# Attention with a gated MLP on one core: the batch loop's turn, the last pair's values and the early MLP products change places

## The chip, the cores and the metric

The kernel runs on one core of a Trainium2 chip. The metric is the device time of one execution in microseconds (us). The time before is the median of three executions.

## What is computed

Four batches, eight heads, 576 positions, head size 64. Queries and keys are rotated by position, each query's softmax over all 576 keys weights the values, and the heads side by side form `x` of 576 x 512. A gated MLP with a convolution over three neighbouring positions follows:

```python
q_rot, k_rot = rotate(q), rotate(k)
scores = scale * np.matmul(q_rot, k_rot.transpose(0, 1, 3, 2))
attn = np.exp(scores - np.max(scores, axis=-1, keepdims=True))
attn = attn / (np.sum(attn, axis=-1, keepdims=True) + 1e-09)
x = heads_side_by_side(np.matmul(attn, v))        # 4 x 576 x 512
h = np.maximum(x @ w_in, 0.0)                     # 4 x 576 x 1024
conv_out = sum(conv_w[k] * shifted(h, k) for k in range(3))
y = (h * sigmoid(conv_out)) @ w_out               # 4 x 576 x 512
```

## The kernel before

Every engine has its own instruction stream, written out by hand, and the streams meet only at semaphores. Each stream has the same frame: a prologue, `attention(0)`, a hardware loop over `b` = 0, 1, 2 whose body is `gated_mlp(b)` and then `attention(b + 1)`, and behind the loop `gated_mlp(3)`. So the loop is entered once by falling into it, turns (jumps back) twice and is left once: four places where attention hands over to the MLP.

**Attention.** Heads go in four pairs. A pair has nine score tiles of 128 query rows (the fifth, i = 4, holds the 64 last rows of both heads), so a batch has 36 tiles t = 0 to 35; the first six are made at the end of the previous MLP. For a tile TensorE writes two halves of 288 scores into PSUM (L337, L338; L332 to L335 for the tail tile), VectorE takes the negated row maximum (L603), ScalarE the exponential with the row sum (L469) into `P`. Tiles go in groups of 2, 2, 1, 2, 2: GpSimd adds epsilon to the group's row sums (L773), VectorE takes the reciprocals (L620), GpSimd multiplies each tile of `P` by them (L752, "normalise"), VectorE transposes it in blocks of 32 into `turned` (L628, "turn"). When all nine tiles of a pair are turned, `times_v` (L365) multiplies by the values in 18 steps of 16 matmuls, cut into five chunks. In the trace each chunk's matmuls stand as L365: 64 records for four steps, 96 for the last six of pair 2, 288 for a whole pair. For pairs 0 to 2 the chunks lie between score tiles of the next pair; the last chunk of pair 2 comes right behind tile 35. The result of a pair lies in four PSUM banks, which ScalarE and VectorE split into a high and a low part (`x_hi` L479, `x_lo` L633). They must be split before the next pair's values may be written there.

**The end of attention before.** On TensorE: `early_hidden` for n = 0 to 3, each nine matmuls (three of the four slices of `x`, which hold pairs 0 to 2; L381 to L383), then the five chunks of the last pair's values, then the loop's turn. ScalarE and VectorE split the last pair at the end of `attention`, ahead of the turn.

**The MLP.** 16 units (two halves of positions, eight slices of 128 hidden features). Unit n: 12 matmuls on TensorE (three where the early part is done), ReLU on ScalarE (L485), first tap (L491), two taps on VectorE (L639), sigmoid (L496), gate (L647), high part (L502), low part on GpSimd (L756), and five units later 12 output matmuls (L397 to L399). A unit's PSUM bank is that of unit n - 4, so `hidden_tile(n)` waits for gate n - 4 from n = 4 on. Beside it VectorE and ScalarE rotate queries and keys of the next batch, whose loads the SyncE queue (SP) issues when the last pair's values are done: V for the next batch's second pair (L256), then `xc` and `xs` (L235, L236). VectorE's first operation on them (L584) stands ahead of its taps of unit 2, so these wait with it. In batch 0 GpSimd also makes the low halves of the weights between tiles (L762), eight times.

VectorE's stream in attention, at tile t: maximum of t, turn of t - 4, reciprocals of the group that ends with tile t - 1. The stretch t = 36 to 39 has only turns, the last reciprocals and the split of pair 2.

Of the kernel before, what the change touches and what calls it, by code (L numbers as in the profile page):

```python
# [5 lines left out]
def rope_attention_conv_gated_mlp(nc, qk, qk_swapped, v_rows, cos_table, sin_table, q_scale,  # L6
# [12 lines left out]
    B, H, _, S = qk.shape  # L19
    D = 64  # L20
    PAIRS = H // 2
    DM, FF = w_in.shape[0] * w_in.shape[1], w_in.shape[2]
    KD = DM // 128
# [12 lines left out]
    AHEAD = FULL + 2  # L36
    NB = S // 32
    BEHIND = 4
    CHUNKS = [(0, 4), (4, 8), (8, 12), (12, 15), (15, NB)]

    ctx = ExitStack()
    with ctx:
# [144 lines left out]
        def tile_at(t):  # L187
            return t // TILES, t % TILES
# [132 lines left out]
        def _(pe):  # L321
# [31 lines left out]
            def times_v(b, pair, chunk):  # L353

                if chunk == 0:
                    pe.wait_ge(turned_done, b * N_SCORES + TILES * (pair + 1))
                    pe.wait_ge(v_in[pair % 2], b * 32 + 16 * (pair // 2 + 1))
                    if pair > 0:
                        pe.wait_ge(x_split, b * PAIRS + pair)
                for k in range(*CHUNKS[chunk]):  # L360
                    for a in range(4):
                        rows = slice(32 * a, 32 * a + 32)
                        for n in range(2):
                            tiles, cols = turned_of(pair, n, a)
                            last = nc.tensor.matmul(banks[n * D:(n + 1) * D, PV0 + a, cols], V[rows, pair % 2, n, k, :],  # L365
                                                    turned[rows, tiles, 32 * k:32 * k + 32],
                                                    start=(k == 0), stop=(k == NB - 1))
                if chunk == len(CHUNKS) - 1:
                    last.then_inc(pv_done, 1)

            def hidden_tile(b, n, ks):


                half, f = n // NF, n % NF
                if n >= 4:
                    pe.wait_ge(gated, b * UNITS + (n - 3))
                cols = slice(half * HALF, half * HALF + HALO)
                fc = slice(f * 128, (f + 1) * 128)
                out = banks[:, n % 4, 0:HALO]
                for k in ks:  # L380
                    nc.tensor.matmul(out, wi_hi[:, k, fc], x_hi[:, k, cols], start=(k == 0), stop=False)  # L381
                    nc.tensor.matmul(out, wi_hi[:, k, fc], x_lo[:, k, cols], start=False, stop=False)  # L382
                    last = nc.tensor.matmul(out, wi_lo[:, k, fc], x_hi[:, k, cols], start=False,  # L383
                                            stop=(k == KD - 1))
                if ks[-1] == KD - 1:
                    last.then_inc(hidden, 1)
# [16 lines left out]
            def attention(b):  # L403
                for t in range(AHEAD, N_SCORES):
                    score(b, *tile_at(t))
                    for pair in range(PAIRS - 1):
                        for chunk in range(len(CHUNKS)):
                            if t == values_at(pair, chunk):
                                times_v(b, pair, chunk)
                for n in range(4):  # L410
                    early_hidden(b, n)
                for chunk in range(len(CHUNKS)):
                    times_v(b, PAIRS - 1, chunk)

            def gated_mlp(b, last):
                pe.wait_ge(x_split, b * PAIRS + PAIRS)
                for n in range(UNITS + LAG):
                    if n < UNITS:
                        hidden_tile(b, n, range(KD) if n >= 4 else range(KD - 1, KD))
                    if n >= LAG:  # L420
                        output_step(b, n - LAG)
                    if not last and UNITS <= n < UNITS + 2:

                        pe.wait_ge(gated, b * UNITS + (UNITS - 2 if n == UNITS else UNITS))
                        score(b + 1, *FIRST_TILES[n - UNITS])
                if not last:
                    for tile in FIRST_TILES[2:]:
                        score(b + 1, *tile)
                    pe.wait_ge(y_copied, 2 * b + 2)

            def early_hidden(b, n):

                pe.wait_ge(exps, b * N_SCORES + N_SCORES - (n < 2))
                if n == 0:
                    pe.wait_ge(x_split, b * PAIRS + (PAIRS - 1))
                    pe.wait_ge(padded, 2)
                    if isinstance(b, int) and b == 0:
                        pe.wait_ge(w_split, H // 2)
                hidden_tile(b, n, range(KD - 1))

            pe.wait_ge(kl_zeroed, 2)
            for tile in FIRST_TILES:
                score(0, *tile)
            attention(0)
            pe.wait_ge(w_split, H)
            with pe.Fori(0, B - 1) as b:
                gated_mlp(b, False)
                attention(b + 1)
            gated_mlp(B - 1, True)


        @block.scalar
        def _(act):
# [56 lines left out]
            def attention(b, first):  # L510
                for t in range(AHEAD - 1, N_SCORES):
                    exp_tile(b, *tile_at(t))
                    for pair in range(PAIRS - 1):
                        if t == values_in(pair):
                            x_high(b, pair)
                    if first and t in WEIGHTS_AT:
                        weights_high(WEIGHTS_AT.index(t))
                load_table(ACT.Sigmoid)
                x_high(b, PAIRS - 1)

            def gated_mlp(b, last):
                for n in range(UNITS + 2):
# [35 lines left out]
            act.wait_ge(rope_lo, H)  # L558
            attention(0, True)
            with act.Fori(0, B - 1) as b:  # L560
                gated_mlp(b, False)
                attention(b + 1, False)
            gated_mlp(B - 1, True)


        @block.vector
        def _(dve):
# [82 lines left out]
            def attention(b):  # L650
                turn(b, 0)
                turn(b, 1)
                for t in range(AHEAD, N_SCORES + BEHIND):
                    if t < N_SCORES:
                        max_tile(b, *tile_at(t))
                    turn(b, t - BEHIND)
                    pair, i = tile_at(t - 1)
                    for k, (_, e) in enumerate(GROUPS):
                        if pair < PAIRS and i == e - 1 and (pair > 0 or k > 2):
                            reciprocals(b, pair, k)  # L660
                    pair, i = tile_at(t)
                    if i == TILES - 1 and pair + 1 < PAIRS:
                        set_tails(b, pair + 1)
                    for pair in range(PAIRS - 1):
                        if t == values_in(pair) + 2:
                            x_low(b, pair)
                x_low(b, PAIRS - 1)

            def gated_mlp(b, last):
                for n in range(UNITS + 2):  # L670
# [59 lines left out]
            dve.wait_ge(consts_in, N_CONSTS)  # L730
            attention(0)
            with dve.Fori(0, B - 1) as b:
                gated_mlp(b, False)
                attention(b + 1)
            gated_mlp(B - 1, True)


# [112 lines left out]
```

## Time and profile before

| | us |
|---|---|
| median of three runs | 601.92 |
| the three runs | 600.47, 601.92, 605.8 |
| the profiled execution, device time | 601.05 |
| its span, first to last instruction | 599.2 |
| TensorE busy | 462.8 (77%) |
| VectorE busy | 421.6 (70%) |
| ScalarE busy | 280.2 (47%) |
| GpSimd busy | 201.0 (34%) |
| TensorE's mean granted clock | 0.906 |

Times in a timeline count from the span's start. A row gives start, duration, engine, line, operation, output and inputs, how many instructions it merges, and in brackets how long the engine stood idle before and what ended that. "issue" is idle time that ends with nothing the profile shows. A clock of 1.00 is 2.4 GHz, 0.50 is 1.2 GHz.

### The profile page before, as it was taken

How to read it: one execution, taken by the hardware profiler on the slowest of the kernel's cores; microseconds unless marked ns; L12 is line 12 of the kernel's file. 1: busy time of each engine (PE TensorE's matmuls, PEld its weight loads, DVE VectorE, ACT ScalarE, POOL GpSimd, SP SyncE). 2: the span in 40 equal slices, each digit the busy share in tenths (PEclk: the TensorE clock that was granted, in tenths of full speed). 3: DMA queues.
4: the chain of work that ended last, by engine and by line, in shares of the span. 5: the costliest groups of instructions: out<-in, count | busy, mean ns of one | idle time of the engine just before them, and what ended most of it. 6: DMA issues, size and time to landing. Idle time of an engine off the chain costs nothing.

```text
span 599.2 us, 17374 instructions
## 1 busy us (share of the span) xinstructions
PE 462.8 (77%) x6784; PEld 414.5 (69%) x6784; DVE 421.6 (70%) x796; ACT 280.2 (47%) x655; POOL 201.0 (34%) x277
## 2 busy tenths in 40 slices
PE   0054868785998698776998699875999698886996
PEld 0043656685998476575998577675999476675996
DVE  6967588707986978815997987824996987834441
ACT  1233555504666445514666453514676454525552
POOL 5312676701321244501431244511432244411321
PEclk9999968888999689987999697986999687988999
DMA  5888122204556111224567110224467101200011
GB/s 197 245 243 269 78 81 81 68 16 166 172 162 178 38 34 61 82 79 156 158 170 184 42 48 38 81 81 164 138 179 186 51 12 73 82 3 1 2 40 40
DMA packets 24370, 62.59 MB, mean 104 GB/s; under 512 B 3296, under 2 KB 7392, under 8 KB 21984
## 3 DMA queue, kind: packets, MB, share of 16 engines
q1 hardware_dynamic: 24288, 61.43, 33.0%
q8 instruction: 59, 0.97, 0.7%
q14 instruction: 23, 0.19, 0.1%
HBM read 42.55 MB, written 4.72 MB: 79 GB/s over the span
## 4 chain that ended last, share of the span: by engine, by line
PE 59%; DVE 13%; issue 13%; DMA 7%; ACT 3%; SPq 2%; POOL 1%; DVEq 1%; ACTq 0%; POOLq 0%
PE banks L365 15%; PE banks L381 6%; PE banks L382 6%; PE banks L383 6%; PE banks L337 6%; PE banks L397 5%; PE banks L399 5%; PE banks L398 5%; DVE neg_max L603 4%; PE banks L338 3%; DVE turned L628 3%; DMA Q<-K 2%; DMA xs<-qk_swapped_dram 2%; DMA KL<-Q 2%; DVE x_lo L633 2%
## 5 line engine op out<-in xcount | busy, mean ns | idle before, releaser
L469 ACT ACTIVATE P<-banks,neg_max 128x576 f32<-128x576 f32 x144 | 106.9, 742 | 132.9 <-DVE neg_max L603 131.3
L337 PE MATMUL banks<-K,Q 128*128 128x288 f32 x256 | 98.5, 395 | 81.1 <-ACT P L469 47.7
L337 PEld LDWEIGHTS banks<-K,Q 128*128 128x128 f32 x256 | 58.6, 229 | 108.7 <-ACT P L469 62.2
L603 DVE TENSOR_REDUCE neg_max<-banks 128x1 f32<-128x576 f32 x144 | 107.2, 747 | 36.2 <-PE banks L338 26.5
L756 POOL TENSOR_TENSOR u_lo<-u,u_hi 128x288 fp32r<-128x288 f32 x64 | 61.1, 956 | 201.5 <-ACT u_hi L502 201.5
L752 POOL TENSOR_SCALAR P<-P,recip 128x576 f32<-128x576 f32 x124 | 91.5, 748 | 69.2 <-DVE recip L620 69.2
L381 PE MATMUL banks<-x_hi,wi_hi 128*128 128x290 f32 x256 | 84.4, 330 | 37.3 <-DVE u L647 12.9
L628 DVE STREAM_TRANSPOSE turned<-P 128x576 f32<-128x576 f32 x144 | 109.5, 765 | 4.1 <-PE banks L365 3.7
L365 PE MATMUL banks<-turned,V 32*64 32x160 f32 (+1 forms) x4608 | 101.2, 303 | 3.6 <-issue 3.6
L639 DVE SCALAR_TENSOR_TENSOR conv<-banks,taps,conv 128x288 f32<-128x288 f32 x128 | 65.7, 514 | 46.0 <-ACT conv L491 45.8
L365 PEld LDWEIGHTS banks<-turned,V 32*64 32x64 f32 x4608 | 81.7, 136 | 15.6 <-issue 15.3
L338 PE MATMUL banks<-KL,Q 128*128 128x288 f32 x256 | 85.0, 342 | 0.0
L381 PEld LDWEIGHTS banks<-x_hi,wi_hi 128*128 128x128 f32 x256 | 54.4, 213 | 41.5 <-DVE u L647 14.6
L382 PE MATMUL banks<-x_lo,wi_hi 128*128 128x290 f32 x256 | 82.2, 321 | 0.0
L383 PE MATMUL banks<-x_hi,wi_lo 128*128 128x290 f32 x256 | 82.1, 321 | 0.0
L397 PE MATMUL banks<-u_hi,wo_hi 128*128 128x288 f32 x256 | 75.9, 296 | 0.0
L398 PE MATMUL banks<-u_lo,wo_hi 128*128 128x288 f32 x256 | 75.7, 296 | 0.0
L399 PE MATMUL banks<-u_hi,wo_lo 128*128 128x288 f32 x256 | 75.7, 296 | 0.0
L338 PEld LDWEIGHTS banks<-KL,Q 128*128 128x128 f32 x256 | 60.4, 236 | 0.0
L382 PEld LDWEIGHTS banks<-x_lo,wi_hi 128*128 128x128 f32 x256 | 54.7, 214 | 0.0
L383 PEld LDWEIGHTS banks<-x_hi,wi_lo 128*128 128x128 f32 x256 | 54.4, 212 | 0.0
L633 DVE TENSOR_TENSOR x_lo<-banks,x_hi 64x64 fp32r<-64x64 f32 (+1 forms) x48 | 16.3, 367 | 51.0 <-ACT x_hi L479 50.8
(50 smaller groups left out, 651.8 us busy)
## 6 DMA issues: line engine op xcount, KB each, us to landing
V<-v_rows_dram SPq DMA_DIRECT2D x16, 1152.0 KB, 5.1
xc<-qk_dram SPq DMA_DIRECT2D x28, 288.0 KB, 2.9
xs<-qk_swapped_dram SPq DMA_DIRECT2D x28, 288.0 KB, 4.2
KL<-Q SPq DMA_DIRECT2D x32, 144.0 KB, 3.6
Q<-K SPq DMA_DIRECT2D x32, 144.0 KB, 3.6
K<-K SPq DMA_DIRECT2D x32, 144.0 KB, 2.6
y_dram<-y_sb SPq DMA_DIRECT2D x8, 576.0 KB, 3.4
wi_raw<-w_in_dram SPq DMA_DIRECT2D x1, 2048.0 KB, 7.8
```

The costliest lines, as they stand in the source:

```text
L337: nc.tensor.matmul(out, Q[:, h, qc], K[:, h, cols], start=True, stop=False)
L338: last = nc.tensor.matmul(out, Q[:, h, qc], KL[:, h, cols], start=False, stop=True)
L365: last = nc.tensor.matmul(banks[n * D:(n + 1) * D, PV0 + a, cols], V[rows, pair % 2, n, k, :], turned[rows, tiles, 32 * k:32 * k + 32], st ...
L381: nc.tensor.matmul(out, wi_hi[:, k, fc], x_hi[:, k, cols], start=(k == 0), stop=False)
L382: nc.tensor.matmul(out, wi_hi[:, k, fc], x_lo[:, k, cols], start=False, stop=False)
L383: last = nc.tensor.matmul(out, wi_lo[:, k, fc], x_hi[:, k, cols], start=False, stop=(k == KD - 1))
L397: nc.tensor.matmul(out, wo_hi[:, f, dc], u_hi[:, n % UR, :], start=(f == 0), stop=False)
L398: nc.tensor.matmul(out, wo_hi[:, f, dc], u_lo[:, n % UR, :], start=False, stop=False)
L399: last = nc.tensor.matmul(out, wo_lo[:, f, dc], u_hi[:, n % UR, :], start=False, stop=(f == NF - 1))
L469: nc.scalar.activation(dst, src, ACT.Exp, bias=neg_max[:, c:c + 1], scale=1.0, accum_out=row_sum[:, c:c + 1]).then_inc(exps, 1)
L603: nc.vector.tensor_reduce(out=neg_max[:, c:c + 1], in_=banks[:, 2 * (t % 2):2 * (t % 2) + 2, 0:HALF], axis=AX.XY, op=ALU.max, negate=True) ...
L628: nc.vector.transpose(turned[:, turned_slot(pair, i), :], p_tile(pair, i)).then_inc(turned_done, 1)
```

## The change

Four edits. The last pair's values move on TensorE out of `attention` into a new function `last_values`, which runs behind the loop's turn and ahead of the early products; there are two of these instead of four (`EARLY = 2`), so n = 2 and 3 are made whole in the MLP. The split of the last pair (`x_high`, `x_low`) moves behind the turn too on ScalarE and VectorE. TensorE's wait for all split weights moves from ahead of the loop into `early_hidden`. On VectorE a group's reciprocals move from behind the turn at the tile after the group's end to behind the maximum of the tile after that; those of the last group stay where they were.

```diff
+    EARLY = 2
@@ tensor
-                for n in range(4):
-                    early_hidden(b, n)
+
+            def last_values(b):
                 for chunk in range(len(CHUNKS)):
                     times_v(b, PAIRS - 1, chunk)
+                for n in range(EARLY):
+                    early_hidden(b, n)
...
-                        hidden_tile(b, n, range(KD) if n >= 4 else range(KD - 1, KD))
+                        hidden_tile(b, n, range(KD) if n >= EARLY else range(KD - 1, KD))
...
                     pe.wait_ge(x_split, b * PAIRS + (PAIRS - 1))
                     pe.wait_ge(padded, 2)
-                    if isinstance(b, int) and b == 0:
-                        pe.wait_ge(w_split, H // 2)
+                    pe.wait_ge(w_split, H)
                 hidden_tile(b, n, range(KD - 1))
...
             attention(0)
-            pe.wait_ge(w_split, H)
             with pe.Fori(0, B - 1) as b:
+                last_values(b)
                 gated_mlp(b, False)
                 attention(b + 1)
+            last_values(B - 1)
             gated_mlp(B - 1, True)
@@ scalar
                 load_table(ACT.Sigmoid)
-                x_high(b, PAIRS - 1)
...
             with act.Fori(0, B - 1) as b:
+                x_high(b, PAIRS - 1)
                 gated_mlp(b, False)
                 attention(b + 1, False)
+            x_high(B - 1, PAIRS - 1)
             gated_mlp(B - 1, True)
@@ vector
                     if t < N_SCORES:
                         max_tile(b, *tile_at(t))
+                    if t == N_SCORES:
+                        turn(b, t - BEHIND)
+                        reciprocals(b, PAIRS - 1, len(GROUPS) - 1)
+                        continue
+                    pair, i = tile_at(t - 2)
+                    for k, (_, e) in enumerate(GROUPS):
+                        if t < N_SCORES and i == e - 1 and (pair > 0 or k > 2):
+                            reciprocals(b, pair, k)
                     turn(b, t - BEHIND)
-                    pair, i = tile_at(t - 1)
-                    for k, (_, e) in enumerate(GROUPS):
-                        if pair < PAIRS and i == e - 1 and (pair > 0 or k > 2):
-                            reciprocals(b, pair, k)
...
-                x_low(b, PAIRS - 1)
...
             with dve.Fori(0, B - 1) as b:
+                x_low(b, PAIRS - 1)
                 gated_mlp(b, False)
                 attention(b + 1)
+            x_low(B - 1, PAIRS - 1)
             gated_mlp(B - 1, True)
```

## Rows read from the trace of the kernel before

**Rows 1.** The page: TensorE's busy time, and the chain that ended last.

```profile
PE 462.8 (77%) x6784; PEld 414.5 (69%) x6784; DVE 421.6 (70%) x796; ACT 280.2 (47%) x655; POOL 201.0 (34%) x277
PE 59%; DVE 13%; issue 13%; DMA 7%; ACT 3%; SPq 2%; POOL 1%; DVEq 1%; ACTq 0%; POOLq 0%
```

**Rows 2.** Timeline, end of batch 1's attention: start, duration, engine, line, work, [idle before].

```profile
250.79 1.91 PE L365 MATMUL banks<-turned,V 32*64 32x160 f32 x96
...
253.48 0.12 DVE L620 RECIPROCAL recip<-recip 128x2 f32<-128x2 f32 x1
...
253.81 1.47 POOL L752 TENSOR_SCALAR P<-P,recip 128x576 f32<-128x576 f32 x2 [0.72 <-DVE recip L620]
254.20 1.02 DVE L633 TENSOR_TENSOR x_lo<-banks,x_hi 128x512 fp32r<-128x512 f32 x3
...
255.25 1.44 DVE L628 STREAM_TRANSPOSE turned<-P 128x576 f32<-128x576 f32 x2
```

**Rows 3.** The same timeline: early products, last values, first turn of the loop.

```profile
255.28 0.61 PE L381 MATMUL banks<-x_hi,wi_hi 128*128 128x290 f32 x1 [2.58 <-DVE x_lo L633]
...
261.58 4.32 PE L365 MATMUL banks<-turned,V 32*64 32x160 f32 x238
266.80 1.24 PE L365 MATMUL banks<-turned,V 32*64 32x160 f32 x50 [0.89 <-issue]
...
272.10 0.60 PE L381 MATMUL banks<-x_hi,wi_hi 128*128 128x290 f32 x1 [4.06 <-issue]
...
273.22 0.40 ACT L485 ACTIVATE banks<-banks 128x290 f32<-128x290 f32 x1 [4.21 <-PE banks L383]
```

**Rows 4.** Timelines: the loop's entry (batch 0), second turn, and exit.

```profile
119.51 1.44 DVE L628 STREAM_TRANSPOSE turned<-P 128x576 f32<-128x576 f32 x2
...
133.48 0.94 ACT L479 ACTIVATE x_hi<-banks 128x512 fp32r<-128x512 f32 x3 [15.24 <-PE banks L365]
...
136.27 0.40 ACT L485 ACTIVATE banks<-banks 128x290 f32<-128x290 f32 x1 [1.85 <-PE banks L383]
...
410.29 0.40 ACT L485 ACTIVATE banks<-banks 128x290 f32<-128x290 f32 x1 [4.67 <-PE banks L383]
...
543.95 0.40 ACT L485 ACTIVATE banks<-banks 128x290 f32<-128x290 f32 x1 [1.85 <-PE banks L383]
```

**Rows 5.** Timeline of ScalarE: the copy that ends each batch's MLP.

```profile
191.36 1.13 ACT L508 ACTIVATE y_sb<-banks 128x1152 f32<-128x1152 f32 x1 [1.17 <-PE banks L399]
...
326.59 1.13 ACT L508 ACTIVATE y_sb<-banks 128x1152 f32<-128x1152 f32 x1 [1.17 <-PE banks L399]
...
463.00 1.13 ACT L508 ACTIVATE y_sb<-banks 128x1152 f32<-128x1152 f32 x1 [1.17 <-PE banks L399]
...
594.31 1.13 ACT L508 ACTIVATE y_sb<-banks 128x1152 f32<-128x1152 f32 x1 [5.60 <-PE banks L399]
```

**Rows 6.** Timelines: the MLP's start behind the entry and behind the exit.

```profile
142.07 1.13 DVE L584 TENSOR_TENSOR xc<-xc,cos_t 128x576 f32<-128x576 f32 x1 [1.56 <-DMA xs<-qk_swapped_dram]
...
144.72 0.41 PE L381 MATMUL banks<-x_hi,wi_hi 128*128 128x290 f32 x1 [2.71 <-DVE u L647]
...
547.83 0.40 PE L381 MATMUL banks<-x_hi,wi_hi 128*128 128x290 f32 x1 [2.70 <-DVE u L647]
```

**Rows 7.** Stages: length, TensorE busy, granted clock, DMA share, GB/s.

```profile
254.00:258.00 4.00, 2.73 (x11) 0.60 0.83 292
119.00:125.00 6.00, 5.42 (x22) 0.50 0.24 101
```

**Rows 8.** Timeline of TensorE: one chunk of values at either clock.

```profile
363.59 2.44 PE L365 MATMUL banks<-turned,V 32*64 32x160 f32 x64
...
369.32 1.37 PE L365 MATMUL banks<-turned,V 32*64 32x160 f32 x64
```

**Rows 9.** Timeline of VectorE in a steady stretch: a maximum, a single tile's reciprocal.

```profile
245.17 0.73 DVE L603 TENSOR_REDUCE neg_max<-banks 128x1 f32<-128x576 f32 x1
...
247.26 0.16 DVE L620 RECIPROCAL recip<-recip 128x1 f32<-128x1 f32 x1 [0.68 <-POOL recip L773]
```

## Prediction, made before the changed kernel ran

> **What bounds the kernel now.** I read the page first: TensorE is busy 77% of the span and carries 59% of the chain that ended last, VectorE 13%, and another 13% is "issue" [rows 1]. So no engine is the bound throughout, and a change of order can only win what TensorE stands idle for on the chain. I then went through the timeline at the four places where attention hands over to the MLP, because the diff moves work there and nowhere else but in VectorE's place for the reciprocals.
>
> Batch 1 shows the pattern. The values of pair 2 end at 250.79 + 1.91 = 252.70. TensorE then stands 2.58 us until pair 2 is split by VectorE (254.20 + 1.02), does 36 early matmuls up to 261.5, writes the last values from 261.58 to 268.04, and stands 4.06 us to 272.10 [rows 2, 3]. What the last values need was there long before: tile 35 is turned at 255.25 + 1.44 = 256.69, and pair 2 split at 255.22 [rows 2]. Of the 4.06 us, some 2.1 are the split of the last pair (0.94 on ScalarE, 1.05 on VectorE, as at the entry [rows 4]); the rest is the loop's turn, since at entry and exit ReLU 0 follows the end of the values by 2.8 us (133.48, where ScalarE starts on them, to 136.27 at the entry), at the turn by 5.2 us (268.04 to 273.22) [rows 3, 4]. The turn thus holds TensorE for at least 4.06 us, of which about 2 lay behind the split.
>
> Behind each hand-over TensorE starves again: it has only short remainders of units 0 to 3 to do and then waits 2.70 us for the gate of unit 1 [rows 6]. The granted clock drops to its lower level (1.2 GHz) after such idle stretches: its mean is 0.60 from 254 to 258 and 0.50 from 119 to 125, each behind an idle wait at the end of pair 2's values [rows 7].
>
> **The change, part by part.** I add up for each hand-over the time up to ReLU 0, and then how long the MLP lasts from ReLU 0 to the copy that ends it.
>
> *A, reciprocals later.* At tile 35 the reciprocals of tiles 32 and 33 now stand behind the maximum of 35, which starts just as the chunk at 250.79 does: 251.65 in place of about 250.2. GpSimd answers 0.33 us after a reciprocal (253.48 to 253.81) and takes 1.47 for two tiles [rows 2], so it is done with 33 at 253.45, and the last epsilon, the last reciprocal (253.85), and the last two normalised tiles (255.65) follow; with turn 33, the split of 1.02 and two turns of 0.72 behind each other VectorE ends at 257.2: 0.5 us later than now. In batch 0 GpSimd also has a weight slice between tiles 32 and 33 and is on the chain throughout; there the whole shift of about 1.6 us goes through, and tile 35 is turned at 119.51 + 1.44 + 1.6 = 122.55 [rows 4]. In the steady stretches I cost the move at nothing. The cover: a reciprocal and the turn that needs it are parted by one turn (0.77) and one maximum (0.73), 1.50 us, and the way through GpSimd takes 0.33 + 0.74 = 1.07 [rows 2, 9]; 0.43 us is spare. The wait of 0.68 us for a single tile's epsilon [rows 9] stays, but then holds a turn and not a maximum; it lies in a stretch where the value chunks set TensorE's pace, so I take no gain.
>
> *B, values straight after the turn.* TensorE reaches the jump at about 252.3 and is ready 4.1 to 4.6 us later, at 256.4 to 256.9. The values can start at 257.3. So the turn is hidden, by the wait for tile 35; the margin is 0.4 to 0.9 us. ScalarE, VectorE and GpSimd jump while nothing needs them for 8 us. The values start 4.3 us earlier than now (261.58), although TensorE's idle time before them grows from 2.58 to 4.6 us.
>
> *C, their length.* Now 6.46 us with one "issue" gap of 0.89 in it [rows 3]. They will meet the low clock that the early products meet now. A chunk takes 2.44 at the low and 1.37 at the full clock [rows 8]; three low microseconds cost 1.4, the entry's five and more cost 2.4. I take 1.8. Directly behind the jump the instruction stream may be thin; of this the rows show only the gap of 0.89 with work in hand and the 4.06 of the jump. I take 0.3 us more at the two turns, near the former, since TensorE waits for tile 35 anyhow, and keep 4.06 for the range.
>
> *D, from the values' end to ReLU 0.* The split of the last pair (0.94 + 1.05 and two hand-offs, 2.1 us) is now covered by 18 early matmuls. A matmul takes (594.31 - 547.83 - 1.6 for a low stretch) / 336 = 0.133 us [rows 5, 6], so they last 2.4, and with the three that finish unit 0 ReLU 0 comes 2.85 after the values. At entry and exit that is what it is now; at the turns it is 5.2 now.
>
> So ReLU 0 comes
> - entry: 122.65 + 6.46 + 1.8 + 2.85 = 133.8, now 136.27: -2.5
> - turns: 257.3 + 6.46 + 1.8 + 0.3 + 2.85 = 268.7, now 273.22: -4.5 each (I take the second like the first)
> - exit: as a turn without the 0.3, against a present without the jump, 268.04 + 2.8: -2.4
>
> *E, the MLP.* From ReLU 0 to the closing copy it takes 55.1 us behind the entry, 53.4 and 52.7 behind the turns and 50.4 behind the exit [rows 3, 4, 5]. Units 2 and 3 are now made whole: 18 matmuls more, 2.4 us, which fit into the 2.70 us of idle time ahead of gate 1 [rows 6]. At the exit that also keeps the clock up: TensorE has 363 matmuls, 48.4 us, and about 0.4 of waiting, in place of 50.4: -1.5. At the entry the tables of the next batch decide. The loads are issued when the values end and land 8.6 us later, at 142.07, with VectorE waiting 1.56 us, and TensorE then 2.71 for gate 2 [rows 4, 6]. That is counted from the values' end, so it stays at the entry. At the turns it is hidden today behind the 5.2 us; with 2.85 in its place the turns get the entry's start. Their MLP becomes 55.1: +1.7 and +2.4. This is the chief giving back.
>
> Sum: entry -2.5; first turn -4.5 + 1.7 = -2.8; second -4.5 + 2.4 = -2.1; exit -2.4 - 1.5 = -3.9. Together -11.3 on the profiled execution's 601.05: 589.8. The median of the runs is 0.9 above that execution, so I say 590.
>
> **The rivals.**
> - *Cheaper start.* The loads land in time at the turns, as they do now, and the low clock costs the lower bound of 1.4. For it: the transfer has the memory to itself there. Against: the entry's row. It gives another 4.1 + 4 x 0.4 = 5.7 us: 584.
> - *The jump starves the values.* They are the densest instruction stream in the kernel: 288 matmuls in 5.6 us, while the MLP, on which the jump falls now, has 12 in 1.6. If a second fetch like the first is exposed inside them, each turn loses 4.06: 8.1 in all, 598. For it: a gap of 0.89 occurs even in straight code, and the load of V is issued in the same moment as the jump. Against: the 0.3 to 0.9 us of waiting and the low clock give the stream time. The Trainium skill, "Runtime: NRT & Kernel Launch", section Instruction fetch mechanics, says that a taken branch breaks the sequential prefetch and forces a fetch before execution can go on; the 4.06 us [rows 3] agree with it, and by that rule the next blocks too would have to come in while the values run.
> - *Slower: the later reciprocals stall VectorE.* If a turn comes to wait for its normalised tile, it is 0.3 us (the 0.73 of the maximum less the spare 0.43) for each of some 16 groups of a batch, 64 in all: +19, so 609 with nothing gained and about 598 with the rest as forecast. It decides once GpSimd's way exceeds 1.50 us. In steady stretches it takes 1.07. In batch 0 with its weights it can happen, eight times at most.
> - *It does nothing.* TensorE could be so bound in the MLP that what is won ahead of it is lost inside. Against it: at the exit nothing stands between MLP and end, and 2.70 us of idle time are there to be filled.
>
> **Chances.** Forecast 0.52 (its own range 587 to 593); cheaper start 0.21; starved values 0.17, mostly in part, 593 to 598; stalls of VectorE 0.05; nothing 0.05. One per cent, 6 us, is about what a measurement of this kernel can tell from no change. Below 595.9 lie the first two and nearly half of the third: 0.81. Slower by over 1% only the fourth with the gains lost: 0.03. The range of 8 in 10 goes from the cheaper start to the starved values: 583.5 to 597.
>
> **What would show it.** In the profile after: the values of the last pair start about 0.1 us behind turn 35 and at most 5 us behind pair 2's values (B); their length is 8 to 9 us with a low clock at their start (C); ReLU 0 comes 2.85 us after them at all four places (D); VectorE's first table product waits 1 to 2 us for a load behind each turn, and TensorE's wait for gate 1 is nearly gone (E); spacing of the maxima in steady stretches unchanged (A). Wrong would be: "issue" gaps of together more than 2 us inside the values at the turns, turns that wait for GpSimd in batches 1 to 3, or no load wait behind the turns.

## The result and the profile after

The changed kernel takes 577.5 us (575.2 to 579.8 in four runs) against 602.2 (the three runs known before and a fourth), a ratio of 0.960 (0.956 to 0.965). The gain is 24.7 us. The direction was forecast; the size was about twice the forecast 12, and 577.5 lies below the range. The profiled execution has a span of 575.7 against 599.2 us. Its page: TensorE's busy time, the chain, and the granted clock in 40 slices:

```profile
PE 456.1 (79%) x6784; PEld 407.9 (71%) x6784; DVE 419.3 (73%) x796; ACT 280.5 (49%) x655; POOL 202.7 (35%) x277
...
PEclk9999979779999597979999597889999789889999
...
PE 51%; DVE 18%; issue 12%; DMA 7%; POOL 4%; ACT 4%; SPq 2%; DVEq 0%; POOLq 0%; ACTq 0%
```

TensorE's work is the same 6784 matmuls, and its busy time fell by 6.7 us [rows 1], since less of it ran at the low clock (96.0 us of the span in place of 112.6 in the two profiled executions). The timeline of the end of batch 1's attention, against [rows 2, 3] (start, duration, engine, line, work, idle time before):

```profile
243.59 1.91 PE L366 MATMUL banks<-turned,V 32*64 32x160 f32 x96
243.70 0.76 DVE L607 TENSOR_REDUCE neg_max<-banks 128x1 f32<-128x576 f32 x1 [0.58 <-PE banks L339]
244.38 0.16 DVE L624 RECIPROCAL recip<-recip 128x2 f32<-128x2 f32 x1
...
247.34 1.02 DVE L637 TENSOR_TENSOR x_lo<-banks,x_hi 128x512 fp32r<-128x512 f32 x3
...
248.39 1.44 DVE L632 STREAM_TRANSPOSE turned<-P 128x576 f32<-128x576 f32 x2
```

```profile
250.10 6.14 PE L366 MATMUL banks<-turned,V 32*64 32x160 f32 x216 [4.60 <-DVE turned L632]
256.63 1.59 PE L366 MATMUL banks<-turned,V 32*64 32x128 f32 x72 [0.39 <-issue]
258.15 0.40 PE L382 MATMUL banks<-x_hi,wi_hi 128*128 128x290 f32 x1
...
259.25 1.06 DVE L637 TENSOR_TENSOR x_lo<-banks,x_hi 128x512 fp32r<-128x512 f32 x3 [9.42 <-ACT x_hi L482]
...
261.26 0.40 ACT L488 ACTIVATE banks<-banks 128x290 f32<-128x290 f32 x1 [2.04 <-PE banks L384]
```

TensorE waits 4.60 us, and what ends that wait is the turned tile 35 (ready at 249.83) and not the jump: at the exit, where no jump lies, it waits 4.38. The loop's turn is no longer on the path. The wait of 4.06 us [rows 3] is gone, and the split of the last pair at 259.25 lies beside early products. The MLP begins 15.8 us behind the end of pair 2's values in place of 20.5.

The copies that end the MLPs, against [rows 5]:

```profile
182.83 1.13 ACT L511 ACTIVATE y_sb<-banks 128x1152 f32<-128x1152 f32 x1 [1.17 <-PE banks L400]
...
312.78 1.13 ACT L511 ACTIVATE y_sb<-banks 128x1152 f32<-128x1152 f32 x1 [1.17 <-PE banks L400]
...
443.77 1.13 ACT L511 ACTIVATE y_sb<-banks 128x1152 f32<-128x1152 f32 x1 [1.18 <-PE banks L400]
...
570.88 1.13 ACT L511 ACTIVATE y_sb<-banks 128x1152 f32<-128x1152 f32 x1 [5.60 <-PE banks L400]
```

The same marks (start of the span or the copy before, the end of pair 2's values, ReLU 0, the closing copy) cut both traces into stages. Lengths in us, before to after; the last column is what the prediction said of the difference:

| stage | batch 0 | batch 1 | batch 2 | batch 3 | sum | predicted |
|---|---|---|---|---|---|---|
| attention up to pair 2's values | 115.7 to 114.1 | 61.3 to 62.7 | 62.6 to 64.1 | 62.7 to 62.8 | +1.4 | 0 |
| from there to ReLU 0 | 20.6 to 17.1 | 20.5 to 15.8 | 21.1 to 15.0 | 18.3 to 14.9 | -17.8 | -13.9 |
| MLP, ReLU 0 to the copy | 55.1 to 51.7 | 53.4 to 51.5 | 52.7 to 51.9 | 50.4 to 49.4 | -7.0 | +2.6 |

The third line holds most of what was missed: 9.6 of 12 us. Two views show what became of it. The clock and TensorE's load in the four MLPs, before and then after (length, busy times, granted clock, DMA share, GB/s):

```profile
136.30:191.20 54.90, 49.15 (x355) 48.44 (x353) 44.92 (x84) 33.68 (x79) 15.24 (x16) 0.97 0.57 171
273.30:326.40 53.10, 49.90 (x354) 48.93 (x354) 45.25 (x84) 33.61 (x79) 16.59 (x16) 0.95 0.55 159
410.30:462.80 52.50, 50.29 (x354) 49.57 (x354) 44.55 (x84) 33.71 (x79) 16.43 (x16) 0.92 0.55 157
544.00:594.20 50.20, 47.50 (x345) 47.09 (x343) 21.11 (x48) 25.06 (x65) 12.88 (x16) 0.97 0.04 13
```

```profile
131.20:182.70 51.50, 50.07 (x373) 49.37 (x372) 44.55 (x84) 33.77 (x79) 16.54 (x16) 1.00 0.60 180
261.30:312.60 51.30, 50.00 (x372) 49.30 (x371) 44.46 (x84) 33.74 (x79) 16.50 (x16) 1.00 0.60 179
391.90:443.60 51.70, 50.38 (x372) 49.44 (x371) 45.11 (x84) 33.61 (x79) 15.97 (x16) 1.00 0.60 178
521.50:570.80 49.30, 48.71 (x363) 48.05 (x361) 21.12 (x48) 25.05 (x65) 12.87 (x16) 1.00 0.04 13
```

All four MLPs now run at 2.4 GHz throughout; before, each had low stretches. With 18 more matmuls in each, TensorE is busy nearly all the time. And VectorE's first table product behind the turn, against [rows 6]:

```profile
265.00 0.51 DVE L643 SCALAR_TENSOR_TENSOR conv<-banks,taps,conv 128x288 f32<-128x288 f32 x1
265.42 0.75 DVE L588 TENSOR_TENSOR xc<-xc,cos_t 128x576 f32<-128x576 f32 x1
```

It follows its predecessor without a gap (0.04 us at the entry). The load wait that the prediction set at three places did not come at any.

### The profile page after: what moved, and what is told of

It reads as the page before. It is cut to its first block, busy times and chain, and to the rows that moved or that the text cites. A ratio compares the mean times of both kernels' runs of the same rounds, so it can differ in the third digit from the quotient of the medians.

```text
span 575.7 us, 17377 instructions
## 1 busy us (share of the span) xinstructions
PE 456.1 (79%) x6784; PEld 407.9 (71%) x6784; DVE 419.3 (73%) x796; ACT 280.5 (49%) x655; POOL 202.7 (35%) x277
## 4 chain that ended last, share of the span: by engine, by line
PE 51%; DVE 18%; issue 12%; DMA 7%; POOL 4%; ACT 4%; SPq 2%; DVEq 0%; POOLq 0%; ACTq 0%
PE banks L366 15%; PE banks L338 6%; DVE neg_max L607 5%; PE banks L398 4%; PE banks L400 4%; PE banks L399 4%; PE banks L382 4%; PE banks L384 4%; PE banks L383 4%; DVE turned L632 3%; PE banks L339 3%; DVE conv L643 3%; DMA Q<-K 2%; DMA xs<-qk_swapped_dram 2%; DVE xs L592 2%
## 5 line engine op out<-in xcount | busy, mean ns | idle before, releaser
L366 PE MATMUL banks<-turned,V 32*64 32x128 f32 (+1 forms) x4608 | 109.9, 322 | 21.6 <-DVE turned L632 20.4
L366 PEld LDWEIGHTS banks<-turned,V 32*64 32x64 f32 x4608 | 90.3, 146 | 33.9 <-issue 29.2
L382 PE MATMUL banks<-x_hi,wi_hi 128*128 128x290 f32 x256 | 77.0, 301 | 3.6 <-DVE u L651 3.6
L384 PE MATMUL banks<-x_hi,wi_lo 128*128 128x290 f32 x256 | 76.0, 297 | 0.0
L383 PE MATMUL banks<-x_lo,wi_hi 128*128 128x290 f32 x256 | 75.9, 297 | 0.0
L382 PEld LDWEIGHTS banks<-x_hi,wi_hi 128*128 128x128 f32 x256 | 48.4, 189 | 6.4 <-DVE u L651 5.5
L384 PEld LDWEIGHTS banks<-x_hi,wi_lo 128*128 128x128 f32 x256 | 48.3, 189 | 0.0
L398 PEld LDWEIGHTS banks<-u_hi,wo_hi 128*128 128x128 f32 x256 | 48.1, 188 | 0.3 <-ACT y_sb L511 0.3
L383 PEld LDWEIGHTS banks<-x_lo,wi_hi 128*128 128x128 f32 x256 | 48.2, 188 | 0.0
```

Of the source, the lines that this page charges most:

```text
L398: nc.tensor.matmul(out, wo_hi[:, f, dc], u_hi[:, n % UR, :], start=(f == 0), stop=False)
```

## Experiments

In the order of the questions: which part carries the gain, whether the load wait is real, and what decides whether it comes.

**The reciprocals alone.** The kernel before with

```diff
-                    turn(b, t - BEHIND)
-                    ... reciprocals of the group that ends with t - 1
+                    ... reciprocals of the group that ends with t - 2
+                    turn(b, t - BEHIND)
```

> The kernel before with the later reciprocals alone. By the prediction (steady stretches unchanged, tile 35 turned 1.6 us later in batch 0 and 0.5 us later in each other batch) it takes about 603 to 605 us against 602. By the theory formed from the trace after (in batch 0 a wait for GpSimd now falls behind a maximum that used to be held up by it, so pair 2 of batch 0 ends 1.6 us earlier, and the rest is as predicted) it takes 600 to 602 us. If the reciprocals carry a large part of the 24 us gained, it takes under 597 us.

Measured: ratio 1.0015 to before (0.998 to 1.005), 602.9 us. No gain and no loss beyond the measurement, which does not tell the first two ranges apart.

**The change without the reciprocals.** The reverse edit on the changed kernel.

> The changed kernel with the reciprocals where they were before. By the prediction it gains 2 to 3 us more than the change: about 575 us. By the theory from the trace after it loses what batch 0 gained: 577.5 to 580 us. Read beside the reciprocals alone: where both differences agree in size, the two parts add up.

Measured: 577.8 us, ratio 0.960 (0.957 to 0.964). Again nothing. The traces show why the sum is about zero. With the late reciprocals pair 2 of batch 0 ends at 114.09 in place of 116.94 us. Over all traces it ends at 112.8 to 115.1 us in the seven traces with the late reciprocals and at 114.4 to 118.8 in the seven with the old ones, 2.4 us apart in the mean. What the traces show as the reason: a maximum now runs ahead of VectorE's wait for a row sum from GpSimd, which is busy with a weight slice; before, it stood behind it (first two lines after, last two before):

```profile
68.84 0.76 DVE L607 TENSOR_REDUCE neg_max<-banks 128x1 f32<-128x576 f32 x1
72.38 0.17 DVE L624 RECIPROCAL recip<-recip 128x1 f32<-128x1 f32 x1 [2.78 <-POOL recip L782]
...
71.80 0.16 DVE L620 RECIPROCAL recip<-recip 128x1 f32<-128x1 f32 x1 [3.02 <-POOL recip L773]
71.88 0.74 DVE L603 TENSOR_REDUCE neg_max<-banks 128x1 f32<-128x576 f32 x1
```

But tile 35 is turned 6.60 us behind it in place of 5.25, and 4.32 in place of 3.99 in the other batches, 2.3 us in all. The prediction had the second half (1.6 and 0.5 us) and not the first.

**Four early products, behind the values.** The changed kernel with

```diff
-    EARLY = 2
+    EARLY = 4
```

> The changed kernel with all four early products behind the last values. If the idle time ahead of gate 1 is what the two whole units fill, ReLU 0 comes 2.4 us later at each of four places and that idle time is back: at least 577.5 + 4 x 2.4 = 587 us, and up to 4 x 1.7 = 7 us more if the granted clock falls in it again (594). If the gain lies in the order alone (values in the wait for the turned tiles), the number of early products does not matter: 578 us. In the profile the first wait of the matmuls of unit 4 is 2.5 us by the first, 0.3 us by the second.

Measured: 588.5 us, ratio 0.978 (0.974 to 0.981). ReLU 0 comes 5.45 to 5.49 us behind the values in place of 3.04 to 3.06, and TensorE again waits for gate 1 (timeline of TensorE behind the first turn):

```profile
272.46 0.40 PE L382 MATMUL banks<-x_hi,wi_hi 128*128 128x290 f32 x1 [2.71 <-DVE u L651]
```

So with the values first, 11 of the 24.7 us hang on the number of early products: what stands behind the values should be as long as the split of the last pair, and the rest fills the wait for gate 1. In the traces 9.7 us lie between the values and ReLU 0. The MLPs, with that wait and 3.4 us of low clock behind it but no load wait, are only 0.4 to 1.0 us longer each.

**The loop's turn alone.** The kernel before, with its order of early products and values kept, but the jump ahead of both and the splits of the last pair behind it on ScalarE and VectorE.

```diff
             with pe.Fori(0, B - 1) as b:
+                last_values(b)      # in this run: four early products, then the values
                 gated_mlp(b, False)
                 attention(b + 1)
```

> The kernel before with the loop's turn ahead of the four early products and the last values, which keep their old order, and the old reciprocals. If the turn's cost of about 2 us behind the split is what is won, it gains 2 x 2.3 = 4.6 us: 597.5 us. If the jump of more than 4 us only takes the place of the 2.58 us wait ahead of the early products, 1.5 to 2 us of that are given back at each of two turns: 600 to 602 us. A gain of 10 us or more would say that the turn is the change.

Measured: 602.8 us, ratio 1.004 (1.000 to 1.008). The early products behind the jump start after 3.46 us of waiting in place of 2.58, and ReLU 0 at the turns comes 2.9 and 3.3 us behind the values, as forecast in D; yet nothing is won. At the first turn the hand-over is no shorter (20.4 us in place of 20.5), since the longer wait is followed by more low clock, in which the early products take 7.5 us in place of 6.3; at the second it is 1.0 us shorter. The MLPs behind the turns are 1.7 and 1.9 us longer, with the following line (VectorE behind the first turn):

```profile
280.94 1.23 DVE L588 TENSOR_TENSOR xc<-xc,cos_t 128x576 f32<-128x576 f32 x1 [1.46 <-DMA xs<-qk_swapped_dram]
```

Here is the load wait that the prediction expected at the turns: 1.46 and 0.89 us, and MLPs of 55.1 and 54.7 us. The prediction's step E described this kernel rightly, and not the one that was forecast.

**The order and the number, without the jump's move.** The kernel before, values ahead of two early products, everything inside `attention`, the jump behind, the old reciprocals.

```diff
+    EARLY = 2
...
-                for n in range(4):
-                    early_hidden(b, n)
                 for chunk in range(len(CHUNKS)):
                     times_v(b, PAIRS - 1, chunk)
+                for n in range(EARLY):
+                    early_hidden(b, n)
...
-                        hidden_tile(b, n, range(KD) if n >= 4 else range(KD - 1, KD))
+                        hidden_tile(b, n, range(KD) if n >= EARLY else range(KD - 1, KD))
```

> The kernel before with the last values ahead of two early products, all of it still inside attention, so that the loop turns behind them; the old reciprocals. Everything of the change but the turn's place and the reciprocals. If the order carries the gain, it takes 577.5 + 2 x 2 (the jump of 4 us is shared between the split's 2 us, which the two early products cover, and the rest) to 577.5 + 2 x 4.3 (the jump lies bare) = 581.5 to 586 us. By the prediction's terms, in which the load wait gives back 4 us at the turns that a bare jump would hide, about 592 us.

Measured: 584.7 us, ratio 0.970 (0.962 to 0.978). The order and the number together bring 17 of 24.7 us without the jump's move. The order alone, with four early products, stands in two runs with the jump ahead (they differ in the reciprocals too, which bring nothing): 602.8 us with the early products first, 588.5 with the values first. Two early products in the old order were not run. In this run the jump is only half bare, TensorE waits 1.29 us for it and 1.74 us for gate 1:

```profile
252.49 6.63 PE L366 MATMUL banks<-turned,V 32*64 32x160 f32 x275 [4.13 <-DVE turned L629]
...
264.08 0.39 PE L382 MATMUL banks<-x_hi,wi_hi 128*128 128x290 f32 x1 [1.29 <-issue]
270.08 0.40 PE L382 MATMUL banks<-x_hi,wi_hi 128*128 128x290 f32 x1 [1.74 <-DVE u L648]
```

Moving the jump ahead of the values brings the other 7, although it brings nothing in the old order.

**Is the load wait behind the entry real?** The kernel before, once more.

> The kernel before once more, for its trace. The prediction took a wait of 1.56 us for a load behind the entry for a fixed price. If it is fixed, VectorE again waits over 1 us there for the load and the MLP behind the entry again takes 55 us from its first ReLU to the closing copy. If it was one execution's accident, the wait is under 0.5 us and the MLP takes about 53 us.

Measured: 602.3 us in one run; VectorE waits 1.55 us (1.56 in [rows 6]), and the MLP behind the entry takes 55.1 us again.

```profile
143.38 1.14 DVE L584 TENSOR_TENSOR xc<-xc,cos_t 128x576 f32<-128x576 f32 x1 [1.55 <-DMA xs<-qk_swapped_dram]
```

It is no accident of one execution.

**The tables' loads first, in both kernels.**

```diff
-                load_v(b + 1, 1)
                 prepare(b + 1)      # its first two heads' loads
+                                    # load_v follows them
```

> The kernel before with the loads of the first two heads' tables of the next batch issued ahead of the load of V. They then land some 2.5 us earlier. If the load wait behind the entry is real and costs what the prediction says, the entry gains 1.6 us of wait and up to 1.7 us of low clock: 599 to 600 us against 602. At the turns nothing changes. If it was an accident: 602 us.

Measured: ratio 0.995 (0.991 to 0.999), 600.3 us. The wait is gone (the load lands 4.2 us behind the values in place of 8.6), and the MLP behind the entry takes 51.8 us in place of 55.1:

```profile
144.12 0.75 DVE L585 TENSOR_TENSOR xc<-xc,cos_t 128x576 f32<-128x576 f32 x1
```

In that stage the wait's price is that of the prediction, 1.6 us plus what follows it, 3.3 together. What follows is the low clock, and 0.4 us by which the product behind the wait is slower (1.13 in [rows 6], 0.75 here). The whole kernel gains 3.2 us by the ratio (0.9 to 5.6), 1.8 by the medians. Against the expectation the MLPs behind the turns are shorter too, 51.9 and 52.0 us; their waits for the load had been 0.35 and 0.41 us.

> The changed kernel with the same loads issued ahead of the load of V. By the trace after, they land just in time (265.29 us for an operation at 265.42 us), so an earlier landing gains nothing: 577.5 us, within 1 us. By the prediction each of three places waits 1.5 us for them and TensorE's clock falls behind it: 577.5 less 3 x 1.5 to 3 x 3.2, 568 to 573 us.

Measured: 576.9 us, ratio 0.960 (0.951 to 0.968): no change. The changed kernel has no wait that could be taken away.

**What brings the load in time?** The load that VectorE waits for is `xs` of the next batch's first head, 288 KB, called the first table here. At the entry it is issued at the same distance behind the values' end in both kernels, 1.69 us. But a DMA queue also brings TensorE's instructions, 57 blocks of 16 KB in the changed kernel by the page's third part. I compared when such a block is fetched and when the first table lands, both in us behind the last values, from the DMA records of the traces:

```
                          first table lands    next fetch for TensorE
before, entry                   8.62                  5.77
before again, entry             8.85                  6.09
turn alone, three places   8.92  8.54  8.36      6.83  6.47  6.32
changed, three places      7.33  7.07  7.05      7.69  7.83  7.79
changed, old reciprocals   7.43  6.97  6.91      7.86  7.87  7.78
changed, four early        7.37  7.34  7.00      7.74  7.81  7.66
```

The two follow each other in every row. That could still be the order of the work in another guise, so I moved the blocks and nothing else:

```diff
+            for _ in range(48):
+                pe.sem_inc(waits_met, 1)
             pe.wait_ge(kl_zeroed, 2)
```

> The changed kernel with 48 semaphore increments ahead of TensorE's first wait, where it stands idle for the loads anyway: nothing changes but where the blocks of its instruction stream, fetched by DMA, begin. In the runs so far the first table's load landed 8.4 to 8.9 us after the last values where a block of TensorE's instructions was fetched 5.8 to 6.8 us after them, and 7.0 to 7.4 us where the next fetch came at 7.7 us or later. If that fetch delays the load, the shift moves it to about 6 us, the load lands at 8.4 us or later, VectorE waits over 1 us at the entry and at both turns, and the MLP behind them takes 53 to 55 us in place of 51.5: 582 to 587 us. If it is the order of the work that brings the load in time, nothing changes: 577.5 us.

Measured: 585.7 us, ratio 0.976 (0.968 to 0.984), 8 us more than the changed kernel. The fetch now falls 5.7, 6.6 and 6.5 us behind the values, and the load lands 8.6, 8.6 and 8.5 us behind them. VectorE behind the first turn, and TensorE, which waits for the gate it has held up:

```profile
270.04 1.36 DVE L590 TENSOR_TENSOR xc<-xc,cos_t 128x576 f32<-128x576 f32 x1 [1.33 <-DMA xs<-qk_swapped_dram]
```

```profile
268.34 0.40 PE L382 MATMUL banks<-x_hi,wi_hi 128*128 128x290 f32 x1 [0.31 <-DVE u L653]
272.91 0.40 PE L382 MATMUL banks<-x_hi,wi_hi 128*128 128x290 f32 x1 [2.68 <-DVE u L653]
```

The three MLPs take 53.5, 55.1 and 54.9 us; those behind the turns have the 55.1 that step E of the prediction gave them, once the blocks lie elsewhere. They are 1.8, 3.6 and 3.0 us longer for waits of 1.27, 1.33 and 1.25 us. Two things add to the wait. TensorE has 3.4 us of low clock behind it at the turns and none at the entry; and one of VectorE's two products behind the wait takes 1.34 to 1.36 us in place of 0.75, where it starts while GpSimd is still at work on `u_lo`. At the first turn (the product is the row of 270.04 above):

```profile
269.99 0.79 POOL L767 TENSOR_TENSOR u_lo<-u,u_hi 128x288 fp32r<-128x288 f32 x1 [20.43 <-ACT u_hi L507]
```

The same shift in the kernel before:

> The kernel before with the same 48 increments. The block boundary moves out of the wait for gate 1 into the end of the last values. If the fetch delays the load, it now lands about 7.3 us after the values at the entry, VectorE's wait there falls from 1.55 us to under 0.4 us and the MLP behind the entry takes 52 to 53 us in place of 55: 599 to 600 us against 602. If not, the wait stays: 602 us.

Measured: ratio 1.004 (1.001 to 1.007), 603.3 us, a miss. The fetch falls 0.85 us behind the values, into the moment in which SyncE issues the loads; the issue of the first table comes 2.7 us behind the values in place of 1.7, the load lands at 10.0, and VectorE waits 2.58 us. SyncE's issues here (first two lines) and before (third), and VectorE here:

```profile
134.65 1.38 SPq L235 DMA_DIRECT2D xc<-qk_dram  x1
136.13 1.67 SPq L236 DMA_DIRECT2D xs<-qk_swapped_dram  x1
...
135.12 0.38 SPq L236 DMA_DIRECT2D xs<-qk_swapped_dram  x1
...
143.48 0.76 DVE L586 TENSOR_TENSOR xc<-xc,cos_t 128x576 f32<-128x576 f32 x1 [2.58 <-DMA xs<-qk_swapped_dram]
```

The turns of the kernel before fit: a fetch of the jump runs from 0.6 to 2.5 us behind the values, and the first table is issued 4.1 and 3.3 us behind them. So a fetch comes with a delay whether it falls on the loads' issue or on their transfer. Which stage of the path the two share was not told apart. The MLP behind the entry takes 54.2 us, less than the 55.1 before in spite of the longer wait; the cause of that stays open.

**What a longer load wait costs.** The changed kernel with one more load between.

```diff
                 load_v(b + 1, 1)
+                sp.wait_ge(spare_in, b * 16)
+                sp.dma_start(spare[:, :, :, :], v_rows[b, 3, :, :, :, :]).then_inc(spare_in, 16)
                 prepare(b + 1)
```

> The changed kernel with one more load of 1152 KB, into memory nobody reads, between that of V and those of the tables. The tables land some 2.8 us later, so VectorE waits 2.5 to 3 us for them at the entry and at both turns. If a load wait costs what the prediction gave it (the wait, and a low clock behind it), each place loses 2.5 to 4.5 us: 585 to 591 us. If the two whole units cover it, since TensorE is the MLP's bound, it loses under 1 us at each: 578 to 580 us.

Measured: 593.7 us, ratio 0.988 (0.982 to 0.995): more than either theory said. The load came later than I had reckoned:

```profile
272.95 0.76 DVE L592 TENSOR_TENSOR xc<-xc,cos_t 128x576 f32<-128x576 f32 x1 [3.72 <-DMA xs<-qk_swapped_dram]
```

The three waits are 4.09, 3.72 and 3.71 us, 11.5 in all, and cost 16 us: 1.4 us for each microsecond of wait. The price is not one number: the 3.9 us of wait in the shifted code cost 8.2, 2.1 for each. The MLPs have 3.4 to 6.8 us at the low clock again. TensorE being full does not cover a late load: it waits 4.5 to 4.9 us for gate 2 there.

**The shifted code with the tables' loads first.** Both edits together.

> The changed kernel with the 48 increments (585.7 us) and the tables' loads issued ahead of the load of V. If the wait for these loads is what the shifted code costs, it is gone, since they land some 3 us earlier wherever the fetch falls: VectorE waits under 0.2 us, the MLPs behind entry and turns take 51.5 to 52 us, 577 to 579 us. If the shift costs by starved values or a luckless clock, it stays at 583 to 586 us.

Measured: 577.1 us, ratio 0.959 (0.952 to 0.966). VectorE's product behind the first turn comes without a gap:

```profile
265.86 0.51 DVE L646 SCALAR_TENSOR_TENSOR conv<-banks,taps,conv 128x288 f32<-128x288 f32 x1
266.29 0.75 DVE L591 TENSOR_TENSOR xc<-xc,cos_t 128x576 f32<-128x576 f32 x1
```

All 8 us are back, although the fetches still fall 5.2 to 6.1 us behind the values. So the shift costs by the load wait; anything else is within the measurement. In the trace of the shifted code the values behind the first turn took 10.2 us in place of 8.1, with 9.1 us at the low clock; at the second turn it was 8.4 in place of 7.4. This version is not faster than the changed kernel beyond the measurement, but with the loads first the shift no longer matters (577.1 us with it, 576.9 without).

## Why the prediction missed

**What bounds the kernel** was read rightly: the gain lies at the four hand-overs and nowhere else.

**A, reciprocals.** Of no account, as forecast, but as a sum of two terms, one of which I had left out. Tile 35 was to be turned 0.5 us later (measured 0.33) and 1.6 later in batch 0 (1.35). That batch 0 reaches that point earlier was missed: I followed the reciprocals to GpSimd and not what the move frees, the maximum in front of which VectorE used to wait. The attention of batches 1 and 2 grew by 1.3 and 1.5 us. With the old reciprocals they take the same (62.7 and 63.7 us, against 62.7 and 64.1 in the changed kernel), so the move of the reciprocals is not the cause. The stretches at the low clock lie elsewhere in each execution.

**B, the values behind the jump.** Right: they start 4.60, 4.55 and 4.38 us behind pair 2 (forecast 4.6), 0.1 to 0.3 us behind the turn of tile 35.

**C, their length.** Forecast 8.3 at the entry, 8.6 at the turns, 8.3 at the exit; measured 7.2, 8.1, 7.4 and 7.4. The mechanism held. The low clock was sized about right: 2.8 to 4.4 us of it fell on the values, which costs half of that, 1.4 to 2.2 us, against the 1.8 taken. Too large was the part for instructions: the "issue" gap of 0.89 us [rows 3] is 0.39, 0.48 and 0.38 behind the turns and at the exit and absent at the entry, so it should not have been kept whole, and 0.3 added to it at the turns. Together with the shorter low stretches in batches 2 and 3 this is 3.5 us of the miss. The rival of starved values, 0.17, did not come.

**D, from the values to ReLU 0.** Right: 3.05 us at all four places against 2.85 forecast; at the turns it was 5.2 and 5.7 before. The split is covered.

**E, the MLP.** This step failed, above all by its claim that the turns get the entry's load wait: +2.6 forecast, -7.0 measured. It has three parts.

- *The load wait.* I took the entry's start [rows 4, 6] as the template for the turns, since the loads' issue is tied to the values' end. The wait at the entry is real and repeats (1.55 us), its price was right, and with the old order it does appear at the turns. But its length was no property of the load. It contained 1.3 us from a fetch of TensorE's instructions that fell on the transfer. Where that fetch falls goes with the order of the work and, as the shifted kernels show, with where the blocks begin. With the early products ahead of the values it came 5.8 to 6.8 us behind them (the kernel before at its entry, the turn alone); with the values first 7.7 to 8.0 (the changed kernel, and the order and the number at the entry). In the changed kernel the load lands at 265.29 us for a product at 265.42, just in time. Shifting the code by 48 idle increments brings the wait back at all three places and costs 8.2 us; issuing the loads first takes it away again. Its absence is 4.1 us not given back at the turns and 3.4 us won at the entry that I had held fixed, 7.5 of the 9.6 us that E missed.
- *The rest at the turns.* These MLPs became 1.9 and 0.8 us shorter than before, where I had them longer. They had 5.4 and 8.3 us of low clock before and none after. Of it, 3.4 us followed the wait for gate 1 at the first turn; the rest had begun ahead of ReLU 0, behind the bare jump. What the clock has cost of the 1.9 and 0.8 us is not shown: with the loads first in the kernel before, the two MLPs took 51.9 and 52.0 us although 6.8 and 7.2 us of each were low, and in the second trace of the kernel before they took 52.6 and 54.9. The Trainium skill, "TensorE: Matmul & The Clock Gate", section HAM oscillation — how this bites in real kernels, says that idle gaps between stretches of matmuls return the clock to its low level time after time; the four MLP rows before (0.92 to 0.97) and after (1.00) agree.
- *The exit.* -0.9 in place of -1.5: gates 1 and 2 hold TensorE for 0.27 and 0.32 us where 0.4 was taken, and its 363 matmuls are busy for 48.7 us where 48.4 was.

The rival "cheaper start" (0.21, 584 us) named the right thing, loads in time and a shorter low clock. It was sized as the return of 1.7 + 2.4 us at the turns and 1.6 for the clock. What it lacked is that the same absence would also free the entry, where the wait existed before. With those 3.4 us, and what C missed beyond these 1.6 (1.9 us), it would have said about 579. The place of the instruction blocks, which decides whether this rival or the forecast comes true, was in neither.

The rival of stalls did not come: with the reciprocals alone there was no loss. Its sum was wrong as well. 19 us on the forecast of 590 give 609, and 19 on the kernel before give 621; the prediction had 598 and 609, the gain taken off twice.

## What to carry to other kernels

The work on which the next dependency hangs should start as soon as its input is there, and independent work belongs into the wait behind it, just as long as that wait: here values first, then two products in place of four, and the other two into the wait for a gate. The loop's jump cost nothing here where the engine waited anyway, and its place alone won nothing in the old order. Where a load lands within a microsecond of its use, issue it earlier before reading anything into a comparison: an edit with no effect on the work, 48 idle increments, moved this kernel by 8 us.

## What the runs showed of the hardware that was not expected

- The place of code in the instruction stream matters for data. A 16 KB fetch for TensorE, which took about 1 us in the DMA records, came with a 288 KB load that landed 1.2 to 1.5 us later (7.1 to 7.3 against 8.5 to 8.6 us behind the values, changed kernel and its shifted code), and this cost the kernel 8.2 us over three places. Falling on the issue instead, it came with an issue 1.0 us later (2.7 against 1.7, at one place).
- A load wait of VectorE at the start of the MLP cost more than its length: 11.5 us of wait 16 us of time, 3.9 us of wait 8.2. TensorE's clock fell behind it (3.4 to 6.8 us low) at five of six places.
- VectorE's product of two inputs of 128x576 took 1.1 to 1.4 us in place of 0.75 where it started while GpSimd made `u_lo`, and 0.76 where that was over (the shifted kernel before, the late loads).
- Values right behind a jump, with 288 matmuls in some 7 us, had no longer "issue" gap in the changed kernel (0.39 and 0.48 us) than without a jump before (0.79 to 0.98 us). Other code around them gave other gaps: two of together 1.26 us in the shifted code with the loads first. TensorE had waited 4.6 us before them and ran at the low clock for their first 4 us (0.50 from 250 to 254 us).

```profile
250.00:254.00 4.00, 3.90 (x120) 3.90 (x126) 0.00 (x0) 0.00 (x0) 0.00 (x0) 0.50 0.08 31
```
